# Decay and state prefix sums of a token-mixer kernel taken in two rounded passes

## The reference

```python
mag = sqrt(a_re**2 + a_im**2)
scale = minimum(mag, 0.999) / (mag + 1e-6)
for t in range(S):                       # S = 768, 8 heads of 48
    S_re, S_im = a_t * (S_re, S_im)      # complex product, a_t scaled as above
    S_re += outer(k_t, v_t)
    y[t] = q_t @ S_re
x = y as (batch, 768, 384)
u = x + (x^T @ U @ V)^T;  x = u + relu(u @ w_ch1) @ w_ch2
theta = x @ w_theta;  y = w_tok_r @ (x cos theta) + w_tok_i @ (x sin theta)
out = (x + y) + relu((x + y) @ w_ch)
```

## Time and profile before

| | before |
|---|---|
| three timed runs | 908.51, 913.71, 913.58 us (median 913.58) |
| the profiled execution's own time | 910.76 us |
| its span | 909.0 us |
| PE busy | 822.3 us (90%), 5424 matmuls |
| DVE busy | 482.6 us (53%) |
| ACT busy | 388.9 us (43%) |
| POOL busy | 265.3 us (29%) |
| mean granted TensorE clock | 0.987 of full speed |

### The profile page before, as it was taken

The page is one execution under the profiler, slowest core; times in us unless marked ns, Lnnn a source line. Parts: engine busy times, 40 slices in busy tenths (PEclk is TensorE's granted clock), DMA queues, the critical chain, the costliest instruction groups (busy, mean ns, idle before and its releaser), DMA issues.

```text
span 909.0 us, 14004 instructions
## 1 busy us (share of the span) xinstructions
PE 822.3 (90%) x5424; PEld 750.1 (83%) x5424; DVE 482.6 (53%) x820; ACT 388.9 (43%) x783; POOL 265.3 (29%) x249
## 2 busy tenths in 40 slices
PE   0359989799999989999999998999999898999998
PEld 0137769789997778999998787998999786999998
DVE  7855538475536636654636544755545552121644
ACT  4756656544333544643323553643322552121321
POOL 7147746642103535120102343220101341020100
PEclk9989999899999999999999999999999999999999
DMA  9401226455643212030244111020064113000161
GB/s 307 161 0 54 62 70 197 134 192 174 236 138 105 72 43 70 1 139 1 107 172 131 53 62 54 17 104 36 13 231 140 53 53 141 1 1 1 49 209 73
DMA packets 43505, 87.61 MB, mean 96 GB/s; under 512 B 6480, under 2 KB 36432, under 8 KB 43440
## 3 DMA queue, kind: packets, MB, share of 16 engines
q1 hardware_dynamic: 43440, 86.72, 28.2%
HBM read 72.55 MB, written 14.16 MB: 95 GB/s over the span
## 4 chain that ended last, share of the span: by engine, by line
PE 76%; DVE 13%; ACT 4%; issue 4%; DMA 2%; POOL 1%; DVEq 0%; POOLq 0%; SPq 0%; ACTq 0%
PE bank L1046 70%; PE bank L1077 2%; PE bank L1083 1%; DVE qk L839 1%; DVE region L847 1%; DMA out<-out_sb 1%; DVE phasor L804 1%; PE bank L1146 1%; PE bank L1231 1%; PE bank L1160 1%; DVE hT L952 1%; DVE phasor L787 1%; DVE logr L783 1%; ACT region L594 1%; DVE phasor L795 1%
## 5 line engine op out<-in xcount | busy, mean ns | idle before, releaser
L1046 PE MATMUL bank<-uT,w_sb 128*128 128x384 f32 x864 | 169.6, 343 | 4.3 <-DVE uT L946 4.3
L1046 PE MATMUL bank<-hT,w_sb 128*128 128x384 f32 x864 | 166.7, 340 | 2.2 <-DVE hT L952 2.2
L1046 PEld LDWEIGHTS bank<-uT,w_sb 128*128 128x128 f32 x864 | 150.9, 188 | 10.3 <-DVE uT L946 4.0
L1046 PE MATMUL bank<-tok,z 128*128 128x384 f32 x864 | 159.1, 338 | 0.0
L1046 PEld LDWEIGHTS bank<-hT,w_sb 128*128 128x128 f32 x864 | 153.0, 190 | 3.8 <-DVE hT L952 3.8
L1046 PEld LDWEIGHTS bank<-tok,z 128*128 128x128 f32 x864 | 149.6, 188 | 0.8
L498 POOL TENSOR_TENSOR kf<-stream,shrink 128x384 f32<-128x384 f32 x24 | 31.5, 1313 | 232.3 <-PE bank L1046 125.7
L952 DVE SCALAR_TENSOR_TENSOR hT<-bank,hT 128x384 fp32r<-128x384 f32 x96 | 52.9, 553 | 71.3 <-ACT hT L646 71.3
L646 ACT ACTIVATE hT<-bank 128x384 fp32r<-128x384 f32 x96 | 46.3, 483 | 91.0 <-PE bank L1046 90.7
L490 POOL TENSOR_TENSOR xs<-x_sb,xs 128x384 fp32r<-128x384 f32 x24 | 25.8, 1090 | 155.0 <-ACT xs L663 155.0
L1046 PE MATMUL bank<-region 96*128 96x128 f32 x384 | 54.5, 287 | 12.0 <-DVE region L847 8.4
(11 more groups left out here) (143 smaller groups left out, 1365.6 us busy)
## 6 DMA issues: line engine op xcount, KB each, us to landing
tok<-w_tok_split SPq DMA_DIRECT2D x48, 768.0 KB, 4.4
w_tok_split<-tok_part SPq DMA_DIRECT2D x24, 384.0 KB, 3.1
stream<-in_q SPq DMA_DIRECT2D x24, 192.0 KB, 2.4
stream<-in_k SPq DMA_DIRECT2D x24, 192.0 KB, 2.6
stream<-in_v SPq DMA_DIRECT2D x24, 192.0 KB, 3.8
w_raw<-in_w SPq DMA_DIRECT2D x12, 384.0 KB, 6.1
stream<-in_w_tok SPq DMA_DIRECT2D x24, 192.0 KB, 3.2
out<-out_sb SPq DMA_DIRECT2D x24, 192.0 KB, 1.9
```

Source lines behind the costliest of these rows:

```text
L1046: return t.matmul(o, lhsT, rhs, start=start, stop=stop, is_transpose=turned)
```

## The change

Each `logr` tile is split into `logr_hi`, its rounded copy in FP32R (new function `round_logr`, ACT), and `logr_lo`, the rest, also FP32R (new function `logr_rest`, POOL). The three masks are copied to FP32R tiles once; zeros and ones stay exact. `sum_decays` becomes two FP32R matmuls and `sum_gains` four. `logr_lo` lies over `logr`; `logr_hi` of chunk 0 lies over `state_sum`, those of the others in three places in turn. Both matmul functions now wait for `logr_lo` of the chunk they need instead of for all of `logr`.

On POOL, the new function, its place behind each `keys` in `batch`, and its place at the end of a batch:

```diff
+            def logr_rest(b, c):
+
+                pool.wait_ge(s_logr_hi.sem, s_logr_hi.at(b, c + 1))
+                g.tensor_tensor(logr_lo[:, c, :], logr[:, c, :], logr_hi(c).bitcast(F32), ALU.subtract)\
+                    .then_inc(s_logr_lo.sem, 1)
...
                     keys(b, c)
                     if b == 0:
                         split(2 * c)
                         split(2 * c + 1)
+                    if c + 2 < C:
+                        logr_rest(b, c + 2)
...
                 if not last:
+                    for c in range(3):
+                        logr_rest(b_next, c)
                     keys(b_next, 0)
```

On ACT, the new function and its calls: at the end of `attention(b, c)`, in the last mixer between `z_high` and `angles`, behind the last `x3_high`, and, in the preparation of the first batch, the masks and the first three chunks:

```diff
+            def round_logr(b, c):
+
+                act.wait_ge(s_logr.sem, s_logr.at(b, c + 1))
+                if b and c:
+                    act.wait_ge(s_mix.sem, s_mix.at(b - 1, 2 * C))
+                if c >= 4:
+                    act.wait_ge(s_gain.sem, s_gain.at(b, c - 2))
+                a.activation(logr_hi(c), logr[:, c, :], ACT.Copy).then_inc(s_logr_hi.sem, 1)
...
                 rows_of_x(b, c)
+                if c + 3 < C:
+                    round_logr(b, c + 3)
...
                 for s in range(2, C):
                     angles(b, s)
                     z_high(b, s)
+                    if s == C - 2 and not last:
+                        round_logr(b_next, 0)
...
                     x3_high(b, n)
+                if not last:
+                    round_logr(b_next, 1)
+                    round_logr(b_next, 2)
...
             act.wait_ge(s_const.sem, CONSTANTS)
+            for exact, mask in ((decay_r, decay_m), (late_r, late_m), (early_r, early_m)):
+                a.activation(exact[:, :], mask[:, :], ACT.Copy).then_inc(s_masks.sem, 1)
...
                 half_angle(0, c)
+            for c in range(3):
+                round_logr(0, c)
```

On DVE, in `next_state`, and on PE, in `sum_decays` and `sum_gains`:

```diff
                 if c == 0:
+                    dve.wait_ge(s_gain.sem, s_gain.at(b, 1))
...
             def sum_decays(b, c):
-                pe.wait_ge(s_logr.sem, s_logr.at(b, C))
+                pe.wait_ge(s_logr_lo.sem, s_logr_lo.at(b, c + 1))
...
-                mm(bank[7][:, 0:D], decay_m[:, :], logr[:, c, :]).then_inc(s_decay.sem, 1)
+                mm(bank[7][:, 0:D], decay_r[:, :], logr_hi(c), stop=False)
+                mm(bank[7][:, 0:D], decay_r[:, :], logr_lo[:, c, :], start=False).then_inc(s_decay.sem, 1)
...
             def sum_gains(b, c):
-                pe.wait_ge(s_logr.sem, s_logr.at(b, C))
+                pe.wait_ge(s_logr_lo.sem, s_logr_lo.at(b, c + 2))
                 pe.wait_ge(s_gain_sb.sem, s_gain_sb.at(b, c))
-                mm(bank[6][:, 0:D], late_m[:, :], logr[:, c, :], stop=False)
-                mm(bank[6][:, 0:D], early_m[:, :], logr[:, c + 1, :], start=False).then_inc(s_gain.sem, 1)
+                mm(bank[6][:, 0:D], late_r[:, :], logr_hi(c), stop=False)
+                mm(bank[6][:, 0:D], late_r[:, :], logr_lo[:, c, :], start=False, stop=False)
+                mm(bank[6][:, 0:D], early_r[:, :], logr_hi(c + 1), start=False, stop=False)
+                mm(bank[6][:, 0:D], early_r[:, :], logr_lo[:, c + 1, :], start=False).then_inc(s_gain.sem, 1)
```

More of the change, by code:

```diff
@@ L68, in token_mixer_program @@
         carry_m = sb("carry_m", [P, P])
+        sums_at = -(-nc.sbuf_base // 32) * 32
         decay_m = sb("decay_m", [P, P])
@@ L71, in token_mixer_program @@
         early_m = sb("early_m", [P, P])
+        decay_r, late_r, early_r = (nc.alloc_sbuf_tensor_at(name, [P, P], F32R, offset=sums_at + i * P * 4)
+                                    for i, name in enumerate(("decay_r", "late_r", "early_r")))
         ident = sb("ident", [P, P])
@@ L74, in token_mixer_program @@
         ln_eps = sb("ln_eps", [P, 1])
+        logr_at = -(-nc.sbuf_base // 32) * 32
         logr = sb("logr", [P, C, D])
+        logr_lo = nc.alloc_sbuf_tensor_at("logr_lo", [P, C, D], F32R, offset=logr_at)
         phasor = sb("phasor", [P, C, 2, D])
@@ L100, in token_mixer_program @@
         state = sb("state", [P, PAIRS, 2, HD])
+        sum_at = -(-nc.sbuf_base // 32) * 32
         state_sum = sb("state_sum", [P, PAIRS, 2, HD])
+        first_hi = nc.alloc_sbuf_tensor_at("first_hi", [P, D], F32R, offset=sum_at)
+        next_hi = nc.alloc_sbuf_tensor_at("next_hi", [P, 3, D], F32R, offset=stream_at + 13 * D * 4)
         flat_state = state[:, :, :, :].rearrange("p j r d -> p (j r d)")
@@ L143, in token_mixer_program, with logr_hi @@
         channel_bank = (bank[0], bank[1], bank[5], bank[4], bank[2], bank[3])
+        def logr_hi(c):
+            return next_hi[:, (c - 1) % 3, :] if c else first_hi[:, :]
         def heads(ap, n=4):
@@ L176, in token_mixer_program @@
         s_logr = sem("s_logr", C)
+        s_masks = sem("s_masks", 0)
+        s_logr_hi = sem("s_logr_hi", C)
+        s_logr_lo = sem("s_logr_lo", C)
         s_quot = sem("s_quot", C)
@@ L542, in _ @@
             quotients(0)
+            for c in range(3):
+                logr_rest(0, c)
             keys(0, 0)
@@ L1327, in _ @@
             pe.wait_ge(s_const.sem, CONSTANTS)
+            pe.wait_ge(s_masks.sem, 3)
             pe.wait_ge(s_zero.sem, 2)
```

## The result

The changed kernel takes 975.57 us (median of four runs, 969.96 to 977.46), the kernel before 912.79 (908.51 to 913.71). The ratio is 1.068, 95% interval 1.063 to 1.073. Forecast were 966, 948 to 982, slower with 0.96. The profiled execution took 975.98 us, 65.2 more than the profiled one of before, and its span is 974.2.

What follows compares the result with a forecast made beforehand. PE was taken to bound the kernel, with 76% of the chain. To 909.0 us of span came 34.8 for stalls net of savings and 19.9 for the clock: 963.7, given as 966, 8-in-10 range 948 to 982.

Steps and rivals of the forecast that it cites:

- The queue wait: Attention, chunks 2 to 4: keys queue behind a subtraction awaiting ACT's rounding after outputs; PE idles 4.8 us, pace 12.9 us.
- PE's own part: PE's time from one chunk's K transposes to the next, without the stall: 8.15 us of the 12.9.
- Chunk 5 comes without a stall: No subtraction stands ahead of keys(5), so the last period is PE's own 8.15 us.
- The sum without the clock: Four batches' added time, 35.7 us, less 0.9 gained by sum_decays in the mixers: 34.8 us more.
- The clock: PE falls to half clock behind each of twelve attention stalls, losing 1.66 us each: 19.9 us in all.
- these matmuls gain nothing, 3.7 at best: sum_decays(1) and sum_gains(0), ahead of the first scores: PE then waits for Q, so no gain counted; bound 3.7 us.
- PE's saving: Shorter FP32R matmuls: sum_decays saves 0.31 us, sum_gains 0.62, at most 19.8 us in all.
- No fall of the clock: Rival: the attention stalls come but PE's clock does not fall; 946 us, chance 0.12.
- POOL at contended prices: Rival: keys at 3.90 us and subtraction at 1.34 add 1.1 to each stall, 13.6 in all; 979 us, chance 0.05.
- Clock low throughout: Rival: PE's clock stays low between stalls, 5.2 us per stall instead of 1.66; 1009 us, chance 0.04.
- The other side: Rival: PE never waits for the subtraction and keeps its 19.8 us saving; 891 us, chance 0.02.
- The edits at nothing: First batch's roundings, mask copies, batch-end roundings and subtractions, and DVE's next_state wait cost nothing; uncovered first roundings 1.5 us once.

Runs made afterwards that it cites:

- filled kernel: The changed kernel plus idle FP32R mask matmuls on PE, 20 ahead of each Kn wait of chunks 2, 3, 4 and 6 ahead of chunk 1's Qn wait: 941.27 us.
- POOL's order moved: The changed kernel with POOL's subtraction for chunk c+1 placed behind keys(c) for chunks 2, 3, 4 instead of ahead of it: 903.16 us, ratio 0.990.
- PE's part alone: The kernel before with only the FP32R matmuls, logs rounded by DVE, low part left out, no added ACT rounding or POOL subtraction in the batches: 902.83 us.
- queue wait alone: The kernel before with only ACT's roundings and POOL's subtractions in the change's places, results unread, PE keeping FP32 matmuls: 984.26 us, ratio 1.080.
- kernel with most fill: The changed kernel with three subtractions a batch behind the keys, plus idle PE matmuls ahead of Qn, first transposes, last second scores and late outputs: 896.37 us.

## Why the prediction was right

**The queue wait.** Each link measured against its term, in the third batch: gains to rows_of_x 1.01 (1.01 expected), rows_of_x to the rounding 0.38 and rounding 0.51 (0.98 expected together), subtraction 0.99 with keys following 0.96 after its start (1.02 expected), keys 544.07 to 547.08 = 3.01 (3.09, the price without DVE beside it), last hand-over 0.05. From rows_of_x to the K transposes it took 547.13 - 542.14 = 4.99, expected 5.29. The pace with the clock held, 12.70, was expected as 12.9; the idle time 4.12 as 4.8. PE's own part, 12.70 - 4.12 = 8.58, took more than the 8.15 I gave it, because its matmuls were not shortened as far as I took (below). So the pace is right in part by luck: a shorter wait and longer work nearly cancel. Chunk 5 comes without a stall, as said.

**The sum without the clock.** Expected 34.8 us. The filled kernel, which still holds both the stalls and the little the fill can delay, lies 28.9 above its before (941.27 - 912.42), and 32.1 with the 3.2 us by which its clock is better than before's. In the traces: 0.39 of PE's work at the lower clock is lost (1.66 of 4.24, as in the prediction), so 37.2 of 95.4 us now and 7.8 of 19.9 before, 29.4 more. Of the 65.2 us between the spans that leaves 35.8 for the rest. The 3.7 between the two readings stay open.

**The clock, mis-sized.** The term was 19.9 us: 1.66 behind each of twelve stalls, and nothing elsewhere. By the traces the clock's part is 29.4, and the 9.5 above the term are most of the 10.5 by which the span, 974.2, exceeds the forecast 963.7. This is the step of the prediction that was off. Behind the twelve stalls themselves PE did 53.1 us of work at the lower clock, 0.39 of which is 20.7: this part was sized rightly, and scores, both transposes and sum_decays took 548.01 to 552.20 = 4.19 there, against 4.24 in the rows I priced by.

What I missed are the other places: 42.3 us of work at the lower clock, against 19.9 before, worth 8.7 us. The largest is attention(0). There the shortened sum_decays(1) and sum_gains(0) make PE wait 1.71 us for Qn of chunk 1, and the clock goes down in all three later batches, on 3.3, 6.5 and 6.5 us of work; before the change it held there in these three (and fell in the first batch, where it now holds). I had written that these matmuls gain nothing, 3.7 at best; they lose. From the K transposes of chunk 0 to those of chunk 5 the third batch takes 586.72 - 524.14 = 62.58 us, against 45.21 before: 17.4 more, where the forecast gave 9.1 + 3 x 1.66 = 14.1. Nearly all of the missing 3.3 is this fall, 0.39 x 6.5 = 2.5, and the 0.7 by which the wait for Qn grew. Three more new falls stand at the start of the matmuls behind the attention stage (143 to 147, 378 to 383, 607 to 611).

The Trainium skill, "TensorE: Matmul & The Clock Gate", section "Why this matters for your kernels", advises against idle gaps between matmul bursts. The trace agrees for the waits of 4.1 us: the lower clock stands behind all twelve. It stands behind waits of 1.7 us as well, though not each time (last section). PE's rows in the third batch, before the first stall and after it:

```profile
530.82 0.64 PE L1126 MATMUL bank<-ident,qk 128*96 128x128 f32 x4 [1.71 <-DVE qk L886]
...
532.79 2.05 PE L1094 MATMUL bank<-region 96*128 96x128 f32 x8 [0.47 <-DVE region L894]
...
552.20 1.17 PE L1094 MATMUL bank<-qk,stream 128*48 128x96 f32 x16
```

**PE's saving, mis-sized too.** It was given as 19.8 at most, 0.93 a chunk: 0.31 for sum_decays and 0.62 for sum_gains. A lone pair of FP32R matmuls holds PE longer than the 0.35 I took from a long row of them: 0.53, of which the first, behind FP32 ones, is 0.26 and the second 0.27. The kernel with POOL's order moved shows it at the full clock:

```profile
508.83 0.60 PE L1132 MATMUL bank<-ident,qk 128*96 128x128 f32 x4
509.18 0.42 PE L1094 MATMUL bank<-next_hi,decay_r 128*128 128x384 f32 x1
509.44 0.34 PE L1094 MATMUL bank<-logr_lo,decay_r 128*128 128x384 f32 x1
509.71 0.87 PE L1094 MATMUL bank<-qk,stream 128*48 128x96 f32 x16
...
512.30 0.59 PE L1197 MATMUL bank<-ident,state 112*96 112x112 f32 x4
...
513.61 0.57 PE L1211 MATMUL bank<-ident,region 112*128 112x112 f32 x4
```

and the kernel before has the transposes of the state ahead of its sum_gains here:

```profile
515.95 0.59 PE L1146 MATMUL bank<-ident,state 112*96 112x112 f32 x4
```

From the K transposes to keys_values it is 0.88, against 1.18 before (513.35 - 512.17); from the transposes of the state to outputs 1.31, against 1.73 (517.68 - 515.95). That is 0.30 and 0.42, and 24 x 0.30 + 20 x 0.42 = 15.6 us in all. The median of PE's part alone shows 9.5 of them. Its fastest run is the profiled one, with 19.2 us of work at the lower clock, about before's 19.9, and it is 14.9 faster than the profiled run of before (910.76 - 895.88). The other three ran at a lower clock, 0.973 to 0.977. So most of what is missing seems to go to the clock; that it is all of it is not shown.

**The rivals.** No fall of the clock (946): near the filled kernel's 941, so this is what the change costs if the clock is held from outside. POOL at contended prices: its last two products took 0.97 each, not 1.24. Clock low throughout: it came back within 7 us of each stall. The other side, 891: not reached even with another order; 903, and 896 with PE kept busy.

**The edits at nothing** held nearly: the first K transposes of all start 0.4 us later (59.51 against 59.14), and the reordered kernel, which still has all roundings and subtractions, has the same median as PE's part alone.

## What to carry to other kernels

A small instruction put into an in-order queue brings all its waits with it: ask what the instruction behind it was free to start on, and follow the chain that it now hangs on, back to the engine that waits. Here 12 x 1 us of work cost 72 us in one place and next to nothing behind the next keys. When one engine's work is shortened, look for the wait that it covered: in this kernel the longer wait for Qn was followed by the lower clock. Idle matmuls in the waits did not shorten them, but took 34 us off the changed kernel by the clock.

## What the runs showed that was not expected

- Short waits were followed by the lower clock as well, but not each time. In the ten kernels' traces, PE waits for Qn of chunk 1 in 40 places. Behind waits of 1.69 to 1.72 us the scores ran at the lower clock in 16 of 17 places, behind 0.98 to 0.99 in 3 of 8 (the kernel before has one, at 69.21; the queue wait alone two), behind 0.80 to 1.31 otherwise in none of 3. Behind the 0.66 to 0.68 that six idle matmuls left, it was none of 12. The one exception among the long ones is in PE's part alone, where the wait at the same place in the two later batches was followed by it:

```profile
282.52 0.64 PE L1088 MATMUL bank<-ident,qk 128*96 128x128 f32 x4 [1.71 <-DVE qk L849]
...
284.49 1.13 PE L1056 MATMUL bank<-region 96*128 96x128 f32 x8 [0.47 <-DVE region L857]
```

So the wait's length alone does not settle it; what else does, no run here shows.

- The spread of one kernel's runs roughly follows the granted clock: PE's part alone ran 895.88, 901.51, 904.15 and 907.13 us at 0.986, 0.975, 0.977 and 0.973. The kernel with most fill ran 894.8 to 898.84 at 0.998 to 0.990. A gain of 1% in such a kernel can hang on where the clock happens to fall.
- POOL's three key products take 3.01 us alone and 3.90 beside DVE's queries; in the stalls they are alone, which makes each stall 0.9 us shorter than the price beside DVE would give.
